# Three Pool instructions instead of six for the low halves of a round's weights

## The reference

```python
a = exp(scores - max); a = a / (sum(a) + 1e-9); x = a @ v      # 8 heads, local window 96 and 8 global keys
h = xt @ U @ V;  u = x + h.transpose(0, 2, 1)
x = u + np.maximum(u @ w_ch1, 0.0) @ w_ch2                     # first feed-forward, 512 -> 2048 -> 512
mixed = np.real(fft(fft(x, axis=1), axis=2));  u = x + mixed
un = (u - mean(u)) / sqrt(var(u) + 1e-6)
out = u + np.maximum(un @ w_ch1, 0.0) @ w_ch2                  # second feed-forward
```

## Time and profile before

| | us |
|---|---|
| three runs, median (lowest to highest) | 683.0 (681.96 to 685.78) |
| the profiled execution | 690.4 |
| its span, first to last instruction | 688.6 |
| PE busy | 663.5 |
| DVE busy | 411.9 |
| Pool busy | 363.4 |
| ACT busy | 329.5 |
| mean granted TensorE clock | 0.983 of full speed |

### The profile page before, as it was taken

The page is one execution under the profiler, slowest core; times in us unless marked ns, Lnnn a source line. Parts: engine busy times, 40 slices in busy tenths (PEclk is TensorE's granted clock), DMA queues, the critical chain, the costliest instruction groups (busy, mean ns, idle before and its releaser), DMA issues.

```text
span 688.6 us, 10390 instructions
## 1 busy us (share of the span) xinstructions
PE 663.5 (96%) x3658; PEld 587.0 (85%) x3658; DVE 411.9 (60%) x952; ACT 329.5 (48%) x722; POOL 363.4 (53%) x375
## 2 busy tenths in 40 slices
PE   7999999999999959999999999999999999999998
PEld 5888888888989848888988988988898889889896
DVE  4777835655543546664587577564876664445454
ACT  4677855534343257443353476442444673443330
POOL 0402336345535199955555876445555965566611
PEclk8899989999999989999999999999999999999999
DMA  7342334112110321212111122112111122212232
GB/s 258 124 152 105 128 146 131 31 62 62 35 59 30 128 84 43 80 61 62 36 58 61 62 62 70 53 62 61 62 60 48 49 90 63 62 61 62 62 122 92
DMA packets 50404, 54.07 MB, mean 79 GB/s; under 512 B 4304, under 2 KB 37200, under 8 KB 50224
## 3 DMA queue, kind: packets, MB, share of 16 engines
q1 hardware_dynamic: 50352, 53.40, 23.8%
HBM read 53.39 MB, written 3.15 MB: 82 GB/s over the span
## 4 chain that ended last, share of the span: by engine, by line
PE 86%; POOL 5%; DVE 4%; DMA 2%; issue 1%; ACT 1%; SPq 0%; DVEq 0%; ACTq 0%; POOLq 0%
PE yP L787 12%; PE yP L789 12%; PE yP L788 11%; PE Yb L766 5%; PE Yb L768 5%; PE Yb L767 4%; PE aP L673 4%; PE Xb L766 3%; PE aP L644 3%; PE Xb L767 3%; PE Xb L768 3%; PE Zb L766 3%; PE Zb L768 3%; PE Zb L767 3%; PE aP L657 2%
## 5 line engine op out<-in xcount | busy, mean ns | idle before, releaser
L533 POOL TENSOR_TENSOR WCL<-w_stage,WCH 128x512 fp32r<-128x512 f32 (+1 forms) x128 | 145.0, 1158 | 172.2 <-ACT WCH L1014 172.1
L1347 DVE TENSOR_TENSOR Y<-yP,Y 128x512 f32<-128x512 f32 x192 | 129.7, 686 | 77.1 <-PE yP L789 76.3
L787 PE MATMUL yP<-WOH,hidH 128*128 128x512 f32 x384 | 154.3, 402 | 11.4 <-DVE Y L1347 10.9
L789 PE MATMUL yP<-WOH,hidL 128*128 128x512 f32 x384 | 152.3, 397 | 0.0
L788 PE MATMUL yP<-WOL,hidH 128*128 128x512 f32 x384 | 152.0, 396 | 0.0
L539 POOL TENSOR_TENSOR WOL<-o_stage,WOH 128x512 fp32r<-128x512 f32 x64 | 81.7, 1299 | 61.8 <-ACT WOH L1021 61.8
L1024 ACT ACTIVATE hidH<-Xb 128x384 fp32r<-128x384 f32 x64 | 31.4, 491 | 146.8 <-PE yP L789 146.8
L787 PEld LDWEIGHTS yP<-WOH,hidH 128*128 128x128 f32 x384 | 72.5, 189 | 28.9 <-DVE Y L1347 15.5
L789 PEld LDWEIGHTS yP<-WOH,hidL 128*128 128x128 f32 x384 | 72.6, 189 | 16.1
L788 PEld LDWEIGHTS yP<-WOL,hidH 128*128 128x128 f32 x384 | 72.6, 189 | 10.8
L766 PE MATMUL Yb<-UCH,WCH 128*128 128x384 f32 x192 | 66.4, 346 | 0.7 <-DVE Xb L1370 0.7
(11 more groups left out here) (213 smaller groups left out, 1303.3 us busy)
## 6 DMA issues: line engine op xcount, KB each, us to landing
w_stage<-w_in SPq DMA_DIRECT2D x128, 128.0 KB, 2.4
o_stage<-w_out SPq DMA_DIRECT2D x32, 512.0 KB, 3.4
V<-v_win SPq DMA_DIRECT2D x8, 704.0 KB, 6.0
K<-k_win SPq DMA_DIRECT2D x8, 644.0 KB, 4.6
Q<-q_t SPq DMA_DIRECT2D x8, 384.0 KB, 3.2
Y<-x_scratch SPq DMA_DIRECT2D x8, 384.0 KB
out<-Y SPq DMA_DIRECT2D x12, 256.0 KB, 3.8
CSraw<-seq_dft SPq DMA_DIRECT2D x1, 1348.0 KB, 5.9
```

The lines of the kernel that those rows point to most:

```text
L533: nc.gpsimd.tensor_tensor(WCL[:, g % 2, u0:u1, :, :], w_stage[:, 1 + u0:1 + u1, :, :], hi32(WCH[:, g % 2, u0:u1, :, :]), ALU.subtract).the ...
L787: nc.tensor.matmul(bank[:, :], hh, WOH[:, h % 2, f, :], start=f == 0, stop=False)
L789: mm = nc.tensor.matmul(bank[:, :], hl, WOH[:, h % 2, f, :], start=False, stop=f == 1)
L1347: nc.vector.tensor_tensor(y, yP[t % 2][:, :], y, ALU.add).then_inc(s_yadd, 1)
```

## The change

`w_lo` makes the seven operands in two instructions (3 operands, 768 columns, then 4 operands, 1024 columns) instead of four, and `o_lo` makes both row blocks in one instruction of 1024 columns instead of two of 512. A round has three of these instructions instead of six. The counts of the semaphores `s_wl` and `s_ol` are halved, and every wait on them with them, so that each waits for the same point of Pool's work as before.

```diff
 def w_load(g):
-    sp.wait_ge(s_wl, 4 * (g - 1) + 2)
+    sp.wait_ge(s_wl, 2 * (g - 1) + 1)
...
 def o_load(g):
-    sp.wait_ge(s_ol, 2 * g)
+    sp.wait_ge(s_ol, g)
...
 def w_sums(g):
-    pool.wait_ge(s_wl, 4 * g)
+    pool.wait_ge(s_wl, 2 * g)
...
 def w_lo(g):
-    for n, (u0, u1) in enumerate(((0, 2), (2, 3), (3, 5), (5, 7))):
-        pool.wait_ge(s_wh, 2 * g + 1 + n // 2)
+    for n, (u0, u1) in enumerate(((0, 3), (3, 7))):
+        pool.wait_ge(s_wh, 2 * g + 1 + n)
         nc.gpsimd.tensor_tensor(WCL[:, g % 2, u0:u1, :, :], w_stage[:, 1 + u0:1 + u1, :, :], hi32(WCH[:, g % 2, u0:u1, :, :]), ALU.subtract).then_inc(s_wl, 1)
...
 def o_lo(g):
     pool.wait_ge(s_oh, g + 1)
-    for f in range(2):
-        nc.gpsimd.tensor_tensor(WOL[:, g % 2, f, :], o_stage[:, f, :], hi32(WOH[:, g % 2, f, :]), ALU.subtract).then_inc(s_ol, 1)
+    nc.gpsimd.tensor_tensor(WOL[:, g % 2, :, :], o_stage[:, :, :], hi32(WOH[:, g % 2, :, :]), ALU.subtract).then_inc(s_ol, 1)
...
 product(g, name):
-    pe.wait_ge(s_wl, 4 * g + 4)
+    pe.wait_ge(s_wl, 2 * g + 2)
...
 out_tile(h, t):
-    pe.wait_ge(s_ol, 2 * (h + 1))
+    pe.wait_ge(s_ol, h + 1)
```

## The result

| | before | after |
|---|---|---|
| median of 12 runs each (lowest to highest), us | 683.69 (681.85 to 685.78) | 686.18 (683.26 to 688.19) |
| ratio, 95% interval | 1 | 1.0031 (1.0016 to 1.0047) |
| span of the profiled execution, us | 688.6 | 683.3 |
| Pool busy, us | 363.4 | 349.6 |

By the ratio the kernel is 2.1 us slower (1.1 to 3.2); the two medians are 2.5 us apart. The forecast was 1.5 us more, and 684.5 as the time. All of this lies within 0.5%, but the interval shows that the change costs time.

A forecast was written before the change was run, and what follows sets the result against it. PE was taken to bound the kernel (busy 663.5 of 688.6 us). Pool's saving of 0.6 us and a hold-up of 2.1 us sum to plus 1.5 us on 683.0, giving 684.5 us, range 681.6 to 687.6.

The forecast's parts named there:

- The bound: Whole kernel: PE busy 663.5 of 688.6 us; cheaper Pool helps only where PE waits for Pool.
- Term 1, the size: Pool's merged instructions: 768 columns take 1.86 us, 1024 take 2.41; 0.38 us less a round.
- Term 1, the worth: Change of batch half, PE's 1.0 us wait for WCL at 276 us: minus 0.6 us, bounds 0 and minus 1.0.
- third rival: Behind each new PE stall the granted clock drops, 3.4 us more: 687.9 us; chance 0.05.
- Term 2, the lock: L1483 at 348 and 494 us waits out Pool's whole 1024-column instruction: 1.12 and 1.0 us, together plus 2.1 us.
- Where it reaches TensorE: Near 348 us: PE stalls some 0.9 us before L5, and P1 starts 1.12 us late.
- The cover at 380 us: At 380.59 and 525.99 us L1483 ends 1.57 us late, but 0.5 us of cover remains; nothing reaches PE.
- the rival in which the cover fails: At 380 and 526 us PE's L4 is delayed, 3.1 us more: 687.6 us; chance 0.11.
- The clock: Rival: half of 3.4 us of work lost behind each new PE stall, 687.9 us; chance 0.05.
- No lock: Rival: DVE gets in within the 1024-column instruction or doesn't meet it; only minus 0.6 remains, 682.4 us; chance 0.16.
- nothing saved: Rival: 1024 columns cost Pool 2.6 us, so no gain and a 2 x 1.3 hold-up, 685.5 us; chance 0.08.
- The sum: Whole kernel: 2.1 - 0.6 = plus 1.5 us, giving 684.5 us; chance 0.60.

The follow-up runs named there:

- second traces: Unchanged kernels profiled again: the kernel before and the full change; stretch from 247 to 302 us 55.89 and 56.04 us.
- second trace with 256 columns: Against the full change, all Pool work in pieces of 256 columns, eleven a round, run twice: 686.53 us, second time 684.78 us.
- the early load: SP loads round 8's weights and round 7's output weights before its mixing-stage wait: 671.80 us on the kernel before, 673.91 us on the full change.
- two passes split: Full change, but output weights in passes 12 and 20 of Pool's 32 are again two instructions of 512 columns: 682.80 us, ratio 0.9988.

## Why the prediction held, and where it was off

- *The bound.* TensorE, with Pool's savings hidden nearly everywhere: right. Pool is 14 us less busy and no stretch got shorter but C.
- *Term 1, the size.* Forecast 1.86 and 2.41 us per instruction, measured 1.851 and 2.400; nearly exact. *Term 1, the worth.* The step that failed is "PE's wait is longer than that, so all of it is gained". In an execution that has TensorE back at full clock early, 0.69 us were gained against 0.63 forecast. Where the low clock lasts 14 us, the saving is hidden behind TensorE's own lateness and is nothing (C 56.04 against 55.89). I took the one trace for the rule, though my third rival rested on the same clock. That the first trace after the change had only 10 us, and so bore out the minus 0.6, was luck.
- *Term 2, the lock.* Forecast 1.12 and 1.0 us at the two places, measured 1.14 and 1.05 (1.09 and 1.25 in the second traces). The longest `UN` was forecast at 2.3 to 2.4 us; it is 2.34 and 2.30 at the two places. That VectorE is held for a whole instruction of 1024 columns, which no row of before could show, is now shown.
- *Where it reaches TensorE.* The new wait before L5 is there, 1.01 us at the weight load and 0.58 at the matmul, against 0.9 forecast (0.93 and 0.50 at the second place); the rest comes at P1, as written.
- *The cover at 380 us.* `UN` 1.67 us late against 1.57 forecast, TensorE not touched, 0.4 us of cover left against 0.5 forecast: right, and with it the rival in which the cover fails is out. The 0.1 us is the small L1472, taken to begin 0.26 us before Pool's end as `UN` does; by the rows of before (it ends at 378.59, Pool's first piece at about 378.56) it is only 0.14. *The clock* is out too: the granted clock is 1.00 from 338 to 356 and from 486 to 498 us after the change, around waits of 0.5 to 0.6 us. Its mechanism is real, though, behind a longer wait: the 2.21 us of the second trace with 256 columns were followed by 3.4 us at half clock. *No lock* is refuted by `UN`'s 2.34 us, *nothing saved* by Pool's 2.40 us where it had 2.6.
- *The sum.* Plus 1.5 where Pool's saving counts (1.50 by the three stretches of the first traces), plus 2.1 to 2.5 where it doesn't (2.14 with the early load, 2.5 by the second traces). Measured in plain runs: 2.1 (1.1 to 3.2). The forecast was 0.6 us low against the middle of that, and the missing part of term 1 is enough to explain it; the interval is too wide to prove that it is the reason. The point of 684.5 also rested on a median of three runs, 683.0, where twelve gave 683.7.

## What to carry to other kernels

Before two instructions of Pool are merged, look at what the gap between them lets in: here 3 of 6 instructions a round were saved, 14 us of Pool time, for a gain of at most 0.7 us and a loss of 2.1 to 2.4. VectorE's tensor_scalar operations from SBUF to SBUF wait here for the whole of the Pool instruction they meet, so the price of a long one is the length it adds (1.1 us here), once at each of the few places where VectorE's queue has no slack, and splitting just those places gives the loss back. And the wait that a list shows first (4.4 and 3.7 us behind a load queued for no reason of its own) was worth 12 us, some five times the question asked.

## What the runs showed of the hardware

- `UN` begins 0.26 us before the recorded end of the Pool instruction that it waited for: seen with 512 columns before; with 1024, it ends 0.29 us after Pool's recorded end, which is 0.25 us less than its own 0.54.
- Even an operation of 2 columns is held (L1472: 0.17 us alone, 0.96 us under a 768-column instruction).
- Not every operation of VectorE from SBUF to SBUF is held. The statistics of a row block (512 columns of `Y`) took 0.68 to 0.70 us in all 12 cases, before and after, though the one below ran wholly within a 768-column instruction of Pool (351.97 to 353.82 us). The small L1478 is a reciprocal and no tensor_scalar; it took 0.15 to 0.17 us in all 6 cases, once at 355.36 us after the change, under the 1024-column instruction that held the `UN` right behind it to 1.53 us.

```profile
352.79 0.70 DVE L1467 BATCH_NORM_STATS2 stat<-Y 128x6 f32<-128x512 f32 x1
```

- A Pool instruction that starts while `UN` still runs takes 0.2 us longer (1.47 against 1.28 us for two equal pieces with two passes split, 0.92 against 0.74 us for L522 behind the long instruction).
- The time at half clock around the same two long waits was 7, 10 or 14 us in different executions of one kernel or its near copies. The 7 us of the first trace of before are two stretches of 3.4 us with full clock between them.
